# Token mixing in a two-part network: hi products of a pair first, a bank for each group of the last batch, turned stores behind token loads

## The reference, cut to what matters

```python
theta = x @ w_theta                        # x: the attention's output, (8, 576, 512)
zr, zi = x * np.cos(theta), x * np.sin(theta)
y = einsum('ts,bsd->btd', w_tok_r, zr) + einsum('ts,bsd->btd', w_tok_i, zi)
u = x + y
x2 = u + np.maximum(u @ w_ch, 0.0)
...
h = np.maximum(x2.transpose(0, 2, 1) @ w_tok1, 0.0) @ w_tok2
u2 = x2 + h.transpose(0, 2, 1)
out = u2 + np.maximum(u2 @ w_ch1, 0.0) @ w_ch2
```

## Time and profile before

| | us |
|---|---|
| median of 3 runs | 1242.36 |
| lowest and highest run | 1239.59, 1243.09 |
| the profiled execution, its own time | 1240.46 |
| its span | 1238.3 |
| PE busy in the span | 1193.1 |

### The profile page before, as it was taken

One profiled execution on the slowest core, in us unless ns is written; L12 is line 12 of the kernel. 1 busy time (PEld: TensorE's weight loads), 2 busy tenths in 40 slices (PEclk: granted clock), 3 DMA queues, 4 the chain that ended last, 5 costly groups with the idle time before them and its releaser, 6 DMA issues.

```text
span 1238.3 us, 20568 instructions
## 1 busy us (share of the span) xinstructions
PE 1193.1 (96%) x7590; PEld 1156.5 (93%) x7590; DVE 842.0 (68%) x1220; ACT 489.2 (40%) x764; POOL 363.2 (29%) x216
## 2 busy tenths in 40 slices
PE   6999999999999999989899899999999989999998
PEld 5899999999899999989798799999999889999998
DVE  3878778686968677686466477676766676666664
ACT  3533324242423323243342355565556533333331
POOL 4442535444342535340444042033112410000000
PEclk9999999999999999999999999999999999999999
DMA  9834445272633450126988767857659999989972
GB/s 260 165 59 94 77 102 88 64 127 38 133 57 84 70 113 0 53 66 221 316 280 290 235 245 268 286 208 281 244 209 327 376 322 291 273 225 305 273 192 51
DMA packets 348428, 228.12 MB, mean 184 GB/s; under 512 B 268880, under 2 KB 316368, under 8 KB 347344
## 3 DMA queue, kind: packets, MB, share of 16 engines
q1 hardware_dynamic: 348368, 227.32, 63.7%
HBM read 136.84 MB, written 92.80 MB: 185 GB/s over the span
## 4 chain that ended last, share of the span: by engine, by line
PE 67%; issue 13%; DVE 9%; POOL 3%; DMA 3%; SPq 2%; ACT 2%; DVEq 0%; POOLq 0%; ACTq 0%
PE bank L42 12%; PE bank L44 12%; PE bank L43 12%; PE bank L1235 9%; PE bank L1237 9%; PE bank L1236 9%; PE bank L260 2%; DVE tokens_cos L649 2%; DMA weights_down<-w_scratch 1%; PE bank L248 1%; POOL weights_rms_inverse L802 1%; POOL tokens_x_token_major L810 1%; DVE weights_fraction L634 1%; DMA g_scratch<-attention_staged 1%; DVE tokens_sin L651 1%
## 5 line engine op out<-in xcount | busy, mean ns | idle before, releaser
L42 PE MATMUL bank<-weights_tok,z_z 128*128 128x288 f32 x576 | 174.5, 303 | 9.0 <-ACT z_z L476 5.7
L43 PE MATMUL bank<-weights_tok,z_z 128*128 128x288 f32 x576 | 170.3, 296 | 0.0
L44 PE MATMUL bank<-weights_tok,z_z 128*128 128x288 f32 x576 | 170.3, 296 | 0.0
L42 PEld LDWEIGHTS bank<-weights_tok,z_z 128*128 128x128 f32 x576 | 108.7, 189 | 12.5 <-ACT z_z L476 7.1
L43 PEld LDWEIGHTS bank<-weights_tok,z_z 128*128 128x128 f32 x576 | 108.9, 189 | 0.0
L44 PEld LDWEIGHTS bank<-weights_tok,z_z 128*128 128x128 f32 x576 | 108.7, 189 | 0.0
L802 POOL TENSOR_TENSOR weights_rms_inverse<-weights_mean_squares,weights_minus_half 128x8 f32<-128x8 f32 x40 | 65.5, 1638 | 135.7 <-DVE weights_mean_squares L596 135.5
L483 ACT ACTIVATE weights_x_channel_major<-attention_u 128x288 fp32r<-128x288 f32 x64 | 28.4, 444 | 146.9 <-DVE attention_u L663 146.9
L817 POOL TENSOR_TENSOR z_z<-tokens_cos,z_z 128x512 fp32r<-128x512 f32 x24 | 34.4, 1435 | 174.9 <-ACT z_z L476 174.9
L42 PE MATMUL bank<-weights_x_channel_major,weights_ch 128*128 128x288 f32 x256 | 77.2, 301 | 0.0
L43 PE MATMUL bank<-weights_x_channel_major,weights_ch 128*128 128x288 f32 x256 | 75.4, 294 | 0.0
(11 more groups left out here) (287 smaller groups left out, 3752.4 us busy)
## 6 DMA issues: line engine op xcount, KB each, us to landing
g_scratch<-attention_staged SPq DMA_DIRECT2D x36, 960.0 KB, 4.6
weights_g<-g_scratch SPq DMA_DIRECT2D x24, 1152.0 KB, 9.1
g_scratch<-attention_staged SPq DMA_DIRECT2D x36, 384.0 KB, 4.5
x_scratch<-attention_u SPq DMA_DIRECT2D x8, 1152.0 KB, 4.5
u_scratch<-attention_u SPq DMA_DIRECT2D x8, 1152.0 KB, 6.2
weights_raw_u<-u_scratch SPq DMA_DIRECT2D x6, 1536.0 KB, 7.6
qkv_u_left<-u_scratch SPq DMA_DIRECT2D x12, 768.0 KB, 9.8
qkv_k<-in_k_dram SPq DMA_DIRECT2D x32, 256.0 KB, 5.0
```

What stands on the lines that cost most here:

```text
L42: eng.matmul(out, w[0], x[0], start=first, stop=False)
L43: eng.matmul(out, w[0], x[1], start=False, stop=False)
L44: return eng.matmul(out, w[1], x[0], start=False, stop=last)
```

## The change

Three edits. In token mixing of pairs, PE first does the hi products (z_hi with both parts of the weights) of the whole pair for all groups, after a wait for a_zhi, and then the lo products, after a wait for g_zlo. In the last batch, which has no attention of a next one, each of the eight groups has a bank of its own: five groups start with pair 0 before the wait for the fourth fraction, two more join after it, seven go together through pairs 1 and 2, then groups 0 to 3 and 4 to 6 finish one set after the other, and group 7, whose bank theta's last tile held, goes alone at the end. In phase b the stores of turned blocks 1 to 3 move from steps 0 to 2 to steps 1 to 3, each behind that step's loads.

```diff
+    ps_tok_last = [*ps_acc, ps_kv, ps_qt, ps_out[1], ps_out[0]]
+
+    def tok_bank(b, g):
+        return ps_tok_last[g] if isinstance(b, int) and b == B - 1 else ps_acc[g % 4]
...
-        def token_mix_step(g, i):
+        def token_mix_hi(b, g, i):
+            half, c = divmod(g, NC)
+            out, x, zt = tok_bank(b, g)[:, 0:HALF], z[0][:, tiles[i], c * P:(c + 1) * P], tiles[i]
+            hs = slice(half * HALF, (half + 1) * HALF)
+            pe.matmul(out, x, wtok[0][:, zt, hs], start=(i == 0), stop=False)
+            pe.matmul(out, x, wtok[1][:, zt, hs], start=False, stop=False)
+
+        def token_mix_lo(b, g, i):
             half, c = divmod(g, NC)
             zt = tiles[i]
-            return split_matmul(pe, ps_acc[g % 4][:, 0:HALF], [x[:, zt, c * P:(c + 1) * P] for x in z],
-                                [w[:, zt, half * HALF:(half + 1) * HALF] for w in wtok],
-                                i == 0, i == NK - 1)
+            mm = pe.matmul(tok_bank(b, g)[:, 0:HALF], z[1][:, zt, c * P:(c + 1) * P],
+                           wtok[0][:, zt, half * HALF:(half + 1) * HALF], start=False, stop=(i == NK - 1))
+            if i == NK - 1:
+                mm.then_inc(p_tok, 1)
+
+        def token_mix_pair(b, pair, groups):
+            pair_tiles = range(2 * pair, min(2 * pair + 2, NK))
+            ready = NK * b + pair_tiles[-1] + 1
+            pe.wait_ge(a_zhi, ready)
+            for i in pair_tiles:
+                for g in groups:
+                    token_mix_hi(b, g, i)
+            pe.wait_ge(g_zlo, ready)
+            for i in pair_tiles:
+                for g in groups:
+                    token_mix_lo(b, g, i)
...
         def token_mix_first_half(b):
             pe.wait_ge(d_frac, NT * b + NJ)
             wait(pe, d_x2, NG * b)
-            for i in range(NK):
-                if i % 2 == 0:
-                    ready = NK * b + min(i + 2, NK)
-                    pe.wait_ge(a_zhi, ready)
-                    pe.wait_ge(g_zlo, ready)
-                for g in range(NC):
-                    mm = token_mix_step(g, i)
-                    if i == NK - 1:
-                        mm.then_inc(p_tok, 1)
+            for pair in range(NT):
+                token_mix_pair(b, pair, FIRST_HALF)
...
+        def token_mix_last():
+            token_mix_pair(B - 1, 0, [0, 1, 4, 5, 6])
+            pe.wait_ge(d_frac, NT * (B - 1) + NJ)
+            token_mix_pair(B - 1, 0, [2, 3])
+            for pair in range(1, 3):
+                token_mix_pair(B - 1, pair, range(NG - 1))
+            for pair in range(3, NT):
+                token_mix_pair(B - 1, pair, FIRST_HALF)
+            for pair in range(3, NT):
+                token_mix_pair(B - 1, pair, range(NC, NG - 1))
+            pe.wait_ge(d_turns, B)
+            for pair in range(NT):
+                token_mix_pair(B - 1, pair, [NG - 1])
...
-            if n == 0:
-                store_last_turned(sp, 1)
-            if n == 1:
-                store_last_turned(sp, 2)
-            if n == 2:
-                store_last_turned(sp, 3)
+            if 1 <= n < NC:
+                store_last_turned(sp, n)
```

More of the change, by code:

```diff
@@ L297, in tensor @@
         tiles = [t for j in range(NJ) for t in (j, NJ + j)] + [2 * NJ]
-        def token_mix_step(g, i):
+        def token_mix_hi(b, g, i):
[5 more added lines that the diff above has]
+        def token_mix_lo(b, g, i):
             half, c = divmod(g, NC)
             zt = tiles[i]
-            return split_matmul(pe, ps_acc[g % 4][:, 0:HALF], [x[:, zt, c * P:(c + 1) * P] for x in z],
-                                [w[:, zt, half * HALF:(half + 1) * HALF] for w in wtok],
-                                i == 0, i == NK - 1)
+            mm = pe.matmul(tok_bank(b, g)[:, 0:HALF], z[1][:, zt, c * P:(c + 1) * P],
[13 more added lines that the diff above has]
+                    token_mix_lo(b, g, i)
+        FIRST_HALF = range(NC)
         def token_mix_first_half(b):
@@ L396, in body @@
                 pe.wait_ge(d_wt, 2 * NT + 1)
-            token_mix_first_half(b)
             if more:
+                token_mix_first_half(b)
                 attend(b + 1, 0)
                 q_transpose(b + 1, 1)
-            for g in range(NC, NG):
-                token_mix(b, g)
-                if more:
+                for g in range(NC, NG):
+                    token_mix(b, g)
                     attend(b + 1, g - 3)
@@ L406, in body @@
                         q_transpose(b + 1, g - 2)
+            else:
+                token_mix_last()
             if first:
@@ L660, in residual @@
                 wait(dve, d_turned, NC * b)
-            dve.tensor_tensor(ug, ps_acc[g % 4][:, 0:HALF], x_half(0, c, half).bitcast(F32), ALU.add).then_inc(d_u1, 1)
+            dve.tensor_tensor(ug, tok_bank(b, g)[:, 0:HALF], x_half(0, c, half).bitcast(F32), ALU.add).then_inc(d_u1, 1)
             dve.wait_ge(d_u1, NG * b + g + 1)
```

## The result

The changed kernel takes 1223.22 us (median of 4 runs, 1220.42 to 1224.31) against 1242.72 us for the kernel before in the same session: a ratio of 0.9845, 95% interval 0.9821 to 0.9868. 1223.5 had been forecast. The profiled execution took 1224.31 us around a span of 1222.2, 16.1 less than the span of before.

The account below looks back on a forecast made before the run. PE, busy 96% of the span, bounds the kernel, so only its stalls can be won: 6.6 + 0 + 5.9 + 5.5 = 18.0 us, giving 1223.5 us. The likeliest case's range is 1219.5 to 1227, the whole range 1219 to 1231.

Parts of the forecast that it names:

- Hi first, loop: Token mixing, six loop batches: waits for z_lo before third and fourth pairs go, 1.10 us a batch, 6.6 in all.
- The cover at the third attention product: Loop: 1.2 us between first norm's end and the third attention product; 0.7 stays after the edit.
- Rival B: Loop gives its gain back at the first attention products: time 1225, or 1230 if the whole chain stays; chance 0.10.
- Batch 0: First batch: PE's 0.9 us earlier start moves into the wait for kv_copy; gain 0, bound a loss of 1.65 us.
- Last batch: Theta to channel mixing: fraction wait 2.60, half clock 1.65, pair waits 1.44 and 0.19 go; sum 5.9 us.
- Rival C: Last batch gives its gain back at channel mixing, DVE behind: gain about 12, time 1229.5; chance 0.06.
- Stores: Next stage: tokens of batch 3 asked for 5 us earlier, stall shrinks from 5.0 to about 1.8 us; 5.5 won.
- The thinnest margin: Next stage: tokens of batch 4 land near 625, half a microsecond before ScalarE wants them.
- Rival A: Token load stays late, held by queue bytes, or tokens 4 take the stall over: gain 12.5, time 1229; chance 0.15.
- Rival D: Slower: lo run changes stationary tile and bank each product; 18.5 ns later each loses all gain, 25 ns gives 1247; chance 0.03.
- The rule weighed: Two-SBUF-input VectorE and SBUF-reading GpSimd instructions exclude each other; 0.9 us here, at most 1.2 us in six batches.
- The base: Gain taken from profiled execution, 1240.46, gives 1222.5; from median of runs, 1242.36, gives 1224.4; 1223.5 chosen between.

Follow-up runs that it names:

- the plain store: Changed kernel plus one extra 288 KB store in long runs to a spare tensor in step 0, where the turned stores had been: 1225.1 us, one run.
- the moved x2 load: Changed kernel with the x2 load of batch 2 moved behind the token load of batch 3: 1223.73 us, ratio 0.9854 to the kernel before.
- the second version beyond the change: Changed kernel plus ScalarE's w_ch split earlier, kv_copy ahead of DVE's w_ch split, turned stores in steps 2 to 4: 1221.46 us, ratio 0.9841.

## Why the prediction was right, point by point

**Hi first, loop: right, size a little low.** 1.22 us a batch, not 1.10. The two restarts after a wait were missed: the second start after each of them came 0.20 us after the first instead of 0.13 (133.04 to 133.24), 0.07 us twice a batch, 0.8 us in six. The cover at the third attention product held: its norm now ends at 149.97 + 0.69 = 150.66 and the product starts at 151.64, 1.0 us, against 1.2 before and 0.7 forecast. Rival B finds no row: no batch of the loop is longer than 67.39 us in any of the ten profiled executions that have the edit. Residual 0 ends 0.8 us before the fifth group starts in batch 1 (141.76 + 0.46 = 142.22 and 143.03; forecast 0.9). That cover is made of the attention products and transposes in between; in the last batch, which has none, hi first alone came 0.32 us late.

**Batch 0: gain 0 right, the loss a matter of chance.** The 0.9 us moved into the wait for kv_copy as forecast (2.55 idle, 2.45 forecast), and kv_copy named as its cause is shown by the two kernels that made it earlier. I took 0 with a bound of 1.65 for half clock. Of the five profiled executions with this gap, two fell to half clock (the changed kernel 76.52, the plain store 76.72) and three did not (hi first alone 75.22, the moved x2 load 75.29, the changed kernel's second profile 75.22).

**Last batch: right.** 6.05 us against 5.9, with the three named rows changed as said; Rival C finds none, channel mixing starts 0.14 us after token mixing and takes 12.58 us as before.

**Stores: right in size, by a hair.** The load was asked for early, landed late, and left 1.73 us of stall (1.8 forecast). "Too short, I take it, for half clock" was the step without ground. Stalls of this load in the versions with the stores moved were followed by half clock at 1.9 (the stores alone), 2.15, 2.28, 2.54 and 2.60 us, the 2.54 in the changed kernel's own second profile, and not at 1.73 (its first), 2.13 and 2.39; so its length alone does not tell. Phase b took 108 to 109 us with half clock, in all but the stores alone; the second version beyond the change took 108.46 without, for its two stalls. The term is 5.3 without half clock and about 3.3 with it (111.63 - 108.35); forecast were 5.5, with 1.9 taken off for a stall given as 1.8. The thinnest margin was named rightly, and was thinner: tokens 4 had 0.03 us, not half a microsecond.

**Rival A.** Its first limb, bytes alone, is refuted by the stores-alone kernel (asked for 4.9 us earlier, 3.1 us less stall). Its second, that the stall goes to tokens 4, does not happen in the changed kernel, but does as soon as tokens 3 come earlier (the moved x2 load): the DMA engines are full there (share 1.05 in the window above), and what one load gains the next gives back.

**Rival D.** The lo run changes stationary tile and bank with each product and keeps its pace: eight L314 products from 132.83 to 133.88, 0.131 us each.

**The rule weighed.** Held by the rows of batch 0 in both directions: DVE's split in first, 2.29 us and GpSimd's z_lo 2.71 instead of 1.30; GpSimd in first, 1.29 us and DVE's split 3.24 instead of 2.29. Neither slows while it holds; the other waits. The Trainium skill, SBUF — State Buffer, section "Who interferes with whom", puts it so: "Issue order, not op shape, decides who blocks." The trace agrees.

**The base.** 1223.5 was taken between the profiled execution's own base and the median's. The medians came to 1223.22 and 1224.91 in two series. That the first lies 0.3 us from the forecast is luck in part: by its profiled executions the change gained 16.1 us of the 18.0 summed up, 1.4 less in batch 0 and 0.8 less in phases c and d with the loop 0.8 better, and by the medians 19.5 and 17.2. What remains open is which executions fall to half clock where, and that decides the last 2 us.

## What to carry to other kernels

Where a product of split values waits for its lo operand, order all hi products of a block of tiles ahead of the lo ones: the time of the hi run is cover that costs nothing, here 2.1 us against a lateness of 0.9. Before an edit moves work forward, look for the next thing that it will wait for and who drives that: in batch 0 kv_copy, driven by another split, took the whole gain. And on an in-order queue that is full, as here, a transfer with short runs belongs behind the load that a compute engine waits for, but each such move shortens the margin of the next load, so read that one too.

## What the runs showed that I had not expected

**The same gap does not always bring half clock.** Behind an idle time of about 2.55 us in batch 0 the granted clock was 0.50 for 3.41 us or stayed at 1.00, in two executions of one program. And the half clock behind a distance of 4.9 to 5.1 us near the start of phase c, which all kernels have, lasted 3.41 us in some executions and 6.83 in others. Phases c and d, which no edit touches, took 539.6 to 539.8 us in five executions and 541.4 to 542.3 in the other eight: in the five, half clock came a second time behind a distance of 2.2 us, some 287 us into phase c, and a later distance was 2.7 us; in the eight it came only behind that later one, which was then 3.9 to 4.0. Executions of one kernel spread by 2.4 to 7.1 us, those of the stores alone by 11.3, so a difference of 1 to 2 us shows in the ledger of stretches and not in the totals. I can't say from these runs what decides it.

**SP's time for a DMA is not its bytes.** 288 KB cost SP 0.43 us as one plain store and 8.24 to 9.19 us as four with runs of 128 bytes; their bytes delayed the load behind them by 0.7 us. Nor is it the runs alone. The four stores of turned block 1 held SP for 8.2 to 9.5 us in the eleven executions that have them in step 0 or 1, and for 4.74 and 4.77 in the two that have them in step 2; those of the other blocks held it for 4.1 to 8.0. So what else the queue holds at that time counts too. How much of it comes from which transfer, no run here separates.
